# Moving the attention pieces of the next chunk through a fused attention and feed-forward pipeline

## The reference

```python
# 1. attention with a decaying state: B=2, H=8, S=768, D=48
for t in range(S):
    cur = einsum('bhd,bhe->bhde', u[None] * kt, vt)
    y[:, :, t] = einsum('bhd,bhde->bhe', rt, state + cur)
    state = w[None, :, :, None] * state + einsum('bhd,bhe->bhde', kt, vt)
# 2. feed-forward: 1536 tokens, 384 -> 2048 -> 384
h = x @ w_in
x2 = where(h > 0, h, exp(minimum(h, 0)) - 1) @ w_out
# 3. eight experts, 384 -> 1024 -> 384, at most 384 tokens each
expert_idx = argmax(x2 @ w_gate, axis=1)      # one expert for each token
out = gate_prob * (maximum(x_e @ w1[e], 0) @ w2[e])   # token goes to its expert's next free slot
```

## Time and profile before

| what | value |
|---|---|
| median of three runs | 422.49 us |
| the profiled execution's own time | 422.56 us |
| its span | 420.7 us |
| PE busy | 410.5 us (98%) |
| PE weight loads busy | 392.6 us (93%) |
| DVE, ACT, POOL busy | 242.8, 188.0, 232.8 us |
| share of PE in the chain that ended last | 84% |
| granted TensorE clock in the slices of the page | 9 in all 40 |

### The profile page before, as it was taken

How to read it: one execution, slowest core, us unless ns; L and a number is a source line. 1 busy time by engine, 2 the same in 40 slices (tenths; PEclk the granted TensorE clock), 3 DMA queues, 4 the chain that set the end, 5 groups by cost and what they waited for, 6 DMA issues and landing times.

```text
span 420.7 us, 9122 instructions
## 1 busy us (share of the span) xinstructions
PE 410.5 (98%) x3539; PEld 392.6 (93%) x3539; DVE 242.8 (58%) x576; ACT 188.0 (45%) x409; POOL 232.8 (55%) x241
## 2 busy tenths in 40 slices
PE   8898999999999999999999999999999999999994
PEld 8798799999999999999999998998999999999994
DVE  7788654484576456645653477686536455464521
ACT  4776453223333332333343455553556445564520
POOL 3788766638657855685563225156082653826531
PEclk9999999999999999999999999999999999999999
DMA  7999967305030403020009001735473936639000
GB/s 267 404 403 407 371 216 282 117 2 154 2 117 12 145 0 118 12 94 2 0 21 338 2 0 39 259 138 182 185 264 111 360 107 253 248 115 363 9 32 28
DMA packets 18649, 64.97 MB, mean 154 GB/s; under 512 B 2203, under 2 KB 11717, under 8 KB 16432
## 3 DMA queue, kind: packets, MB, share of 16 engines
q1 hardware_dynamic: 16816, 59.68, 39.0%
q0 software_dynamic: 1792, 4.73, 2.9%
HBM read 51.98 MB, written 13.21 MB: 155 GB/s over the span
## 4 chain that ended last, share of the span: by engine, by line
PE 84%; DVE 5%; issue 4%; POOL 3%; ACT 2%; POOLq 0%
PE bank L1352 24%; PE bank L1354 23%; PE bank L1353 23%; PE bank L1370 3%; POOL g_lo L700 2%; PE bank L1452 1%; DVE wd_lo L1050 1%; PE bank L1434 1%; PE bank L1438 1%; PE bank L1398 1%; PE bank L1672 1%; DVE elu L1180 1%; PE bank L1427 1%; ACT elu L856 1%; PE bank L1430 1%
## 5 line engine op out<-in xcount | busy, mean ns | idle before, releaser
L700 POOL TENSOR_TENSOR g_lo<-elu,g_hi 128x256 fp32r<-128x256 f32 x95 | 72.2, 760 | 94.0 <-ACT g_hi L863 93.4
L1352 PE MATMUL bank<-xt,wd_hi 128*128 128x256 f32 x285 | 80.9, 284 | 2.0 <-DVE elu L1180 1.8
L1354 PE MATMUL bank<-xt,wd_lo 128*128 128x256 f32 x285 | 80.4, 282 | 0.0
L856 ACT ACTIVATE elu<-elu 128x256 f32<-128x256 f32 x96 | 40.1, 418 | 90.1 <-DVE elu L1172 89.6
L1353 PE MATMUL bank<-xt,wd_hi 128*128 128x256 f32 x285 | 80.3, 282 | 0.0
L1180 DVE SCALAR_TENSOR_TENSOR elu<-elu,bank 128x256 f32<-128x256 f32 x96 | 40.4, 421 | 50.5 <-ACT elu L856 50.4
L1352 PE MATMUL bank<-wd_hi,g_hi 128*128 128x392 f32 (+1 forms) x192 | 68.3, 356 | 0.3 <-ACT x2row L824 0.3
L1353 PE MATMUL bank<-wd_lo,g_hi 128*128 128x392 f32 (+1 forms) x192 | 65.2, 339 | 0.0
L1354 PE MATMUL bank<-wd_hi,g_lo 128*128 128x392 f32 (+1 forms) x192 | 65.1, 339 | 0.0
L863 ACT CAST g_hi<-elu 128x256 fp32r<-128x256 f32 x96 | 39.0, 406 | 43.3 <-DVE elu L1180 43.2
L1172 DVE TENSOR_SCALAR elu<-bank 128x256 f32<-128x256 f32 x80 | 33.7, 422 | 41.9 <-PE bank L1354 40.9
(11 more groups left out here) (220 smaller groups left out, 951.5 us busy)
## 6 DMA issues: line engine op xcount, KB each, us to landing
we_raw<-wexp SPq DMA_DIRECT2D x8, 1536.0 KB, 6.5
wd_raw<-wexp SPq DMA_DIRECT2D x8, 1536.0 KB, 6.6
rkt<-rkt SPq DMA_DIRECT2D x12, 512.0 KB, 5.5
nat<-nat SPq DMA_DIRECT2D x9, 672.0 KB, 4.1
xrow<-slots SPq DMA_DIRECT2D x16, 193.0 KB, 7.2
wd_raw<-win SPq DMA_DIRECT2D x4, 768.0 KB, 9.2
wd_raw<-wout SPq DMA_DIRECT2D x4, 768.0 KB, 9.3
wo_tr<-wouttr SPq DMA_DIRECT2D x1, 3072.0 KB, 16.4
```

The source lines that it names most:

```text
L700: nc.gpsimd.tensor_tensor(g_lo[:, f % 4, :], elu[:, f % 2, :], g_hi[:, f % 4, :].bitcast(F32), ALU.subtract).then_inc(s_glo, 1)
L856: nc.scalar.activation(elu[:, f % 2, :], elu[:, f % 2, :], ACT.Exp, scale=-1.0 if n == 0 else 1.0).then_inc(s_exp, 1)
L1352: mm(dst, w_hi, x_hi, start=start, stop=False)
L1354: return mm(dst, w_lo, x_hi, start=False, stop=stop)
```

## The change

`plan` takes the place of the four helpers and gives each piece of each chunk a step of its own. `meeting(c)` is the step of chunk c's `scores`: 0/2, 0/9, 1/0, 1/6, 1/13 for chunks 2 to 6, then 2/3, 2/11, 3/3, 3/11, 4/3. From chunk 4 on, `outer`, `back`, `state` and `x_lo` of chunk c stand at the meeting of chunk c+1, behind its `scores`. PE's part of a meeting is `fc1`, `scores(c+1)`, `outer(c)`, `back(c)`, `fc2`. Chunks 2 and 3 keep their steps, but `state` moves ahead of the weight piece in DVE's queue. Masks stand one and two steps behind the scores from chunk 5 on. `route` moves later, by one or two steps, and `logits` ahead of `scores` in step 1/6. `w_in_hi(1)` moves ahead of `x_hi(1)`, `w_in_lo(1, ...)` ahead of `x_lo(1)` and of step 0/0's L1180, and POOL's `keys(2)` waits for both halves of it. ACT copies a block's x2 (L824) before step 2's L863. In block 5 `expert0_lo` stands between L1172 and L1180. One of 14 matmuls ahead of the start is left out.

```diff
-        WARM = 14
+        WARM = 13
...
-                            (6, 7, 8, 8, 9, 10) if n == 0 else (3, 5, 6, 7, 8, 9)))
+                            (7, 8, 9, 10, 11, 11) if n == 0 else
+                            (3, 6, 7, 8, 9, 12) if n < NB - 2 else (3, 5, 6, 8, 9, 10)))
...
+        def meeting(c):
+
+            return {2: 2, 3: 9, 4: FT, 5: FT + 6, 6: 2 * FT - 3}.get(c, 2 * FT + 3 + 8 * (c - 7))
+
+        def plan(c):
+
+            b, before = meeting(c), meeting(c - 1)
+            steps = {"scores": b, "decay": b + (2 if c > 4 else 0), "keys": before + 1, "queries": before + 2,
+                     "mask0": b + (c == 2 or c > 4), "mask1": b + 1 + (c == 2 or c > 4)}
+            if c == 2:
+                steps.update(diagonal=2, natural=3, outer=6, state=6, back=7, low=8)
+                del steps["keys"], steps["queries"]
+            elif c < 5:
+                steps.update(rk=before + 3, with_u=before + 4, sum=before + 5, diagonal=before + 5, natural=before + 6)
+                if c == 3:
+                    steps.update(outer=11, state=11, back=13, low=14)
+            else:
+                steps.update(rk=b - 2, with_u=b - 1, sum=b, diagonal=b, natural=b + 4)
+            if c == 6:
+                steps.update(rk=b - 4, with_u=b - 3)
+            if c == 7:
+                steps.update(rk=b - 3)
+            if c > 3:
+                steps.update(outer=meeting(c + 1), state=meeting(c + 1), back=meeting(c + 1), low=meeting(c + 1))
+            return steps
...
 (POOL, before the loop)
-            pool.wait_ge(s_wlo, 1)
+            pool.wait_ge(s_wlo, 2)
             keys(2)
...
 (ACT, before the loop)
             x_hi(0)
+            w_in_hi(1)
             x_hi(1)
-            w_in_hi(1)
...
 (ACT, in a step)
+                    if n and f == LAG - 1:
+                        x2_rows(n - 1)
                     act.wait_ge(s_g, q + 1)
                     nc.scalar.copy(g_hi[:, f % 4, :], elu[:, f % 2, :]).then_inc(s_ghi, 1)
-                    if n and f == LAG - 1:
-                        x2_rows(n - 1)
...
 (DVE, before the loop)
             x_lo(0)
+            w_in_lo(1, 0)
+            w_in_lo(1, 1)
             x_lo(1)
-            w_in_lo(1, 0)
...
 (DVE, in a step)
-                    if n == 0 and f == 0:
-                        w_in_lo(1, 1)
...
+                    if n == NB - 1 and f >= F_E0:
+                        expert0_lo(f - F_E0)
                     dve.wait_ge(s_exp, q + 1)
                     V.scalar_tensor_tensor(out=elu[:, f % 2, :], ...
+                    c = chunk_for("state", n, f)
+                    if c is not None and c < 4:
+                        state(c)
...
+                    c = chunk_for("sum", n, f)
+                    if c is not None and c > 4:
+                        sum_bonus(c)
                     for j in range(2):
-                        c = mask_at(n, f, j)
+                        c = chunk_for(f"mask{j}", n, f)
...
+                    c = chunk_for("low", n, f)
                     if c is not None:
                         x_lo(c)
+                    c = chunk_for("state", n, f)
+                    if c is not None and c > 3 and leaves_state(c):
+                        state(c)
...
 (PE, in a step)
                     fc1(n, f)
-                    c = chunk_at(n, f, 0)
+                    if n == 1 and f == F_LG:
+                        logits()
+                    c = chunk_for("scores", n, f)
                     if c is not None:
                         scores(c)
...
-                    c = is_at(n, f, OUTER)
+                    c = chunk_for("outer", n, f)
                     if c is not None and leaves_state(c):
                         outer(c)
-                    c = is_at(n, f, BACK)
+                    c = chunk_for("back", n, f)
                     if c is not None:
                         back(c)
```

More of the change, by code:

```diff
@@ L327, in build, with chunk_for @@
         NTAB = 1
[L329 to L337, removed]
-                    return c
-            return None
[L341 to L359, removed]
+        def meeting(c):
[20 more added lines that the diff above has]
+            return steps
+        PLANS = {c: plan(c) for c in range(2, NSTEP)}
+        def chunk_for(what, n, f):
+            for c, steps in PLANS.items():
+                if steps.get(what) == FT * n + f:
+                    return c
+            return None
         def score_banks(c):
@@ L682, in ahead @@
             def ahead(n, f):
-                if n == 0 and f in (2, 3):
-                    (diagonal, natural_k1)[f - 2](2)
-                c = chunk_at(n, f, 0)
+                c = chunk_for("diagonal", n, f)
+                if c is not None:
+                    diagonal(c)
+                c = chunk_for("decay", n, f)
                 if c is not None and has_state(c) and leaves_state(c):
                     decay_state(c)
[L689 to L692, removed]
+                for what, piece in (("natural", natural_k1), ("keys", keys), ("queries", queries), ("rk", raw_bonus),
+                                    ("with_u", with_u)):
+                    c = chunk_for(what, n, f)
+                    if c is not None and (what != "natural" or leaves_state(c)):
+                        piece(c)
             for n in range(NB):
@@ L1027, in state @@
                 if c >= 2:
-                    dve.wait_ge(s_y, c)
+                    dve.wait_ge(s_y, c + (c > 3))
                 u = u_bank(c).rearrange("p (h e) -> p h e", h=HP)
@@ L1097, in shift @@
                     dve.wait_ge(s_lg, 1)
+                    dve.wait_ge(s_xhi, 10)
                     L = ps_lg.rearrange("p (t e) -> p t e", t=BT)
@@ L1187, in _ @@
                         split_lo(f, 1)
+                    c = chunk_for("sum", n, f)
+                    if c is not None and c > 4:
+                        sum_bonus(c)
                     for j in range(2):
-                        c = mask_at(n, f, j)
+                        c = chunk_for(f"mask{j}", n, f)
                         if c is not None:
                             mask(c, j)
[L1192 to L1196, removed]
+                    c = chunk_for("low", n, f)
                     if c is not None:
                         x_lo(c)
-                    c = chunk_at(n, f, 5)
-                    if c is not None and c + 1 < NSTEP:
-                        sum_bonus(c + 1)
+                    c = chunk_for("state", n, f)
+                    if c is not None and c > 3 and leaves_state(c):
+                        state(c)
+                    c = chunk_for("sum", n, f)
+                    if c is not None and c < 5:
+                        sum_bonus(c)
                     if n and f == LAG - 1:
@@ L1215, in _ @@
                         gated_lo()
-                    if n == NB - 1 and f >= F_E0:
-                        expert0_lo(f - F_E0)
                     if n == NB - 1 and f == F_A:
@@ L1387, in outer @@
             def outer(c):
-                pe.wait_ge(s_k1n, c + 1)
+                pe.wait_ge(s_k1n, n_states(c + 1))
                 if c < 2:
@@ L1394, in outer @@
                     pe.wait_ge(s_xlo, 2 * c)
+                    pe.wait_ge(s_z, n_states(c))
                 for hp in range(HP):
@@ L1413, in back @@
                     pe.wait_ge(s_xlo, 2 * c)
-                    pe.wait_ge(s_z, n_states(c + 1))
+                    pe.wait_ge(s_z, n_states(c + 1 if c < 4 else c))
                     wait_if(pe, s_row, (c - 3) // 2)
@@ L1546, in logits @@
                 pe.wait_ge(s_gw, 16)
-                pe.wait_ge(s_xlo, 10)
+                pe.wait_ge(s_xlo, 8)
                 for t in range(BT):
@@ L1588, in _ @@
                             x2_transpose(t)
-                    if n == 1 and f == F_LG:
-                        logits()
                     if n and f == route(n - 1)["count"]:
```

## The result

The changed kernel takes 418.11 us (417.85 to 418.64, 4 runs), the one before 422.56 us (421.98 to 422.76, 4 runs) beside it: a ratio of 0.9900, 95% interval 0.9888 to 0.9911, or 4.4 us less. The forecast was 418.8. The profiled execution took 418.15 us, its span is 416.3.

What follows compares the result with a forecast made beforehand. PE, busy 98% of the span, bounds the kernel; real waits stand only at 0/2, 0/7 and block 5. Terms -1.5 - 0.3 - 1.1 - 0.3 - 1.0 + 0.5 = -3.7 take 422.5 to 418.8 us, range 417.1 to 421.3.

Steps and rivals of the forecast that it cites:

- Fewer borders: PE, blocks 1 to 4: broken steps fall from 18 to 10 at 0.2 us each, -1.5 us (0.8 to 1.6).
- POOL's k: Steps 2/0 and 2/8: PE's two 0.25 us waits for POOL's natural k shrink or go, -0.3 us.
- Block 0: Both waits of PE in block 0 and the dropped warm-up matmul together: -1.1 us (0.4 to 2.0 saved).
- the first wait: Step 0/2: PE's 1.36 us wait for DVE's combine; start about 1.2 us sooner, some waited for again at 0/6.
- The second wait: Step 0/7: the way back's 1.1 us wait for the state; state product ahead of the weight piece gives 0.68 us.
- the WARM edit: Start of the kernel: one warm-up matmul of 0.44 us fewer, given 0.1 us (0 to 0.44).
- Block ends: Step 5/3: fc2's 0.3 us wait for ACT's x2 copy goes, -0.3 us (0 to 0.3); hidden in blocks 2 to 4.
- Block 5: DVE's expert weight splits fill its gap, cutting PE's waits for the combine: -1.0 us (-1.3 to +0.5).
- Block 1: Routing meets chunk 5's masks, making DVE late around step 1/8: +0.5 us of PE (0 to 2.0).
- The rest at nothing: Meetings and loads: ACT's, DVE's, POOL's and SP's other work stays covered, costing PE 0 us.
- Rival D: Meetings: DVE's in-order queue is the bound, seven stalls of 0.8 us make it slower, 424.4 us; chance 0.06.
- Rival A: Blocks 0 and 5 keep their waits, POOL's backlog and ACT's casts setting the pace: 420.3 us; chance 0.17.

Runs made afterwards that it cites:

- experiment 3: Changed kernel with way back, its copies and state one step behind the meeting from chunk 6 on: 419.33 us.
- experiment 5: Changed kernel with the order of weight pieces in block 0's first steps as before: 418.54 us.
- experiment 6: Changed kernel with DVE's state product of chunks 2 and 3 again behind the second weight split in block 0: 419.22 us.
- experiment 10: Changed kernel with block 0's count one step later, plus either chunk 2's masks a step later (418.35 us) or 14 warm-up matmuls, not 13 (418.43 us).
- experiment 7: Changed kernel with ACT's copy of the finished block's x2 again behind g_hi of its step: 419.17 us.
- experiment 4: Changed kernel with the first expert's weight splits in block 5 again at the end of the step, behind the combine: 419.65 us.
- Experiment 8: Changed kernel with block 0's routing (logits to gates) begun one step earlier, 420.27 us; or with only its count one step later, at 1/11, 418.44 us.
- experiments 9: Changed kernel with the later chunks' pattern carried into block 0, chunk 2's outer product, state and way back at step 0/9: 418.57 us.

## Why the prediction was right

**The total** came out 0.7 lower than forecast. The mechanisms hold, with block 1's wait only half in its place, and the sizes err in both directions. Start and block 0 gave 0.6 where 1.1 was forecast, blocks 1 to 4 1.7 for 1.3, block 5 1.9 for 1.3, the part behind it 0.2 for nothing. The forecast had 1.2 too little in three places and 0.5 too much in one; that they offset one another is luck.

1. **Fewer borders, -1.5: right.** 0.21 a break in the earlier trace rows is 0.21 after, and 0.22 where a break is put back (experiment 3). The choice that the inner border is free (1.5 and not 0.8) is shown by the 0.62 of step 3/3. The Trainium skill (TensorEngine Tiling (Array Packing), Key Properties) says that changing the mode drains the engine; the trace agrees at the outer borders and shows nothing of it between the tiled forms.
2. **POOL's k, -0.3: right.** Both waits are gone; block 2 fell by 0.76, which is two breaks and 0.36.
3. **Block 0, -1.1: the mechanism right, the size 0.2 too large.** From its first `fc1` it is -0.92. The mis-sized term is the 0.4 by which POOL and DVE were to be ahead at 0/7: the first wait gave 1.1 and took 0.85 back (experiment 5), now a wait for L1057 ahead of 0/6, so 0.23 is left of it. The warning that some is waited for again at 0/6 was right in place and too small. The second wait gave the 0.68 worked out from the earlier trace rows (0.7, experiment 6), and 0.4 of that wait stays. "Behind it PE never waits again in block 0" held: there is no wait of PE from 0/8 on. The 0.1 for the WARM edit is worth nothing (experiment 10). Then the execution began 0.32 later, which nothing ties to the change (last section).
4. **Block ends, -0.3: right in place, mis-sized.** It is 0.45 in block 5 (experiment 7), above the bound of 0.3 that I gave it: the wait is 0.31, and the late `fc2` also restarts 0.1 late. What I did not see: with the shifted plan block 1 would have needed it too, 0.36 at step 1/3.
5. **Block 5, -1.0: mis-sized.** The stretch gave 1.87, of which 0.45 is item 4's and 1.4 this one's (experiment 4), just past the bound of -1.3. I kept 0.3 for a wait for ACT's cast. DVE does wait for it, as a row of all waits in block 5 of the changed kernel shows, but ahead of the combine, where it has that time, and PE waits for nobody in block 5:

```profile
DVE we_lo L1164 <- ACT we_hi L853: 3.3, 5, 1.1
```

   With item 4 it makes 0.6, the largest single difference between forecast and result.
6. **Block 1, +0.5: right in size, and the place only half.** Block 1 is 44.54, where 43.43, 1.09 more scores and two breaks less (0.4) make 44.12: it pays 0.4, and in most other executions 0.9. PE stands at 1/10 ahead of `count`, which needs `choose`, and not at `fc1`. Experiment 8 shows that both are late together: take one away and the other stands at its full length.
7. **The rest at nothing: right.** After no meeting does PE wait. Rival D, DVE's queue at the meetings, did not come in.

Of the signs named ahead, block 3 was to be shorter by 0.4 and is by 0.52; block 4 by 1.51, of which 1.09 is one chunk's scores, which stand in block 1 now; the sums had that, the sentence had not. The combine of step 0/0 was to be near 18 us: 18.34. The wait for the state was to be half or less: 0.4 of 1.1. Block 5 near 35.5: 34.85. Rival A came in part: PE waits again in block 0, ahead of 0/6, for a weight piece of DVE. Whether POOL's backlog sets the pace there is open.

Two slips of the working change nothing: the chances of the forecast, A and B add up to 0.89 and not 0.88, and six borders at 0.1 leave 0.9 of item 1's 1.5 and not 0.8.

What stays open: whether block 0 is bound by POOL's own 36 of 44.7 us or by what the two engines cost each other. The experiments moved work of both and changed the sum by 0.1; none took work away from either.

## What to carry to other kernels

Count what a stream on a full engine pays for being broken, put the pieces of other shapes behind one another, and check from start to start that the inner borders are free. A piece whose operands come from an engine that idles in fixed gaps belongs into the gap, not behind the result that others wait for: that one move was worth nearly as much as eight breaks. Where two engines hold each other up and both are full, a wait that is moved away can come back a few steps on: of the wait ahead of 0/2, 0.85 of 1.1 us stood again ahead of 0/6, and experiments 9 and 10 moved waits by one or two steps and won next to nothing, while the 0.7 of experiment 6 stayed won. Compare at a step further on before you call it won.

## What the runs showed of the hardware

A DVE instruction of 8 or 16 columns takes 0.17 us. With two inputs in SBUF it took 0.75 and 0.92 when it started 0.03 and 0.3 us behind a POOL instruction (L1117 and L1120 above). The Trainium skill (SBUF — State Buffer, Who interferes with whom) says that a DVE instruction with two inputs in SBUF and a GpSimd instruction that reads SBUF exclude one another, and that the later one blocks until the other is through; the two agree with it. The reduction L1119, 0.1 us behind POOL's L648, still took 0.17. The cast L1103 has one input and was held all the same: 0.74 in ten of the eleven profiled executions that have it at step 1/7 beside POOL's L707, 0.02 us behind it in the one shown, and 0.16 in the changed kernel's, 0.03 behind it. The same section of the skill counts casts among the operations that can take both ports, and lets the order of issue decide who blocks; the trace does not contradict that, but why the order fell differently in the one execution stays open. So a tiny operation that is held is as dear beside POOL as a full one, and one such cast is a matter of 0.6 us from one execution to the next.

The first load of the chain also varies. The chain of waits of the changed kernel begins with it, while that of the kernel before begins with the warm-up:

```profile
2.21 5.70 DMA rkt<-rkt
7.93 0.69 DVE prod L1005
```

In the fourteen profiled executions that second product of DVE (L1005) began between 7.43 and 8.29 us and the first `fc1` between 15.62 and 16.35, always 8.06 to 8.38 us behind it, whatever the kernel. So the start moves the whole kernel by up to 0.7 us from one execution to the next, and differences below that between two single profiles are to be read from a later step on. The expert work behind does the same: from step 5/15 to the end it takes 155.84 to 156.67 us in the fourteen, though no edit touches it.
